# Retention in a fused block: the product with the states takes both heads of a pair at once, from a block-diagonal matrix

## The reference

```python
scores = scale * np.matmul(q, k.transpose(0, 1, 3, 2))      # q, k, v: (4, 8, 576, 64)
Dmat = np.where(rel >= 0, gamma[:, None, None] ** rel[None, :, :], 0.0)
ret = scores * Dmat[None, :, :, :]
attn_out = np.matmul(ret, v)
...
xn = x / rms * rms_g                                        # x: (2304, 512)
g = xn @ w_gate; val = xn @ w_val                           # d_ff 1536
x = (g * (1.0 / (1.0 + np.exp(-g))) * val) @ w_out
...
h = x @ w_in                                                # d_ff 2048
out = np.where(h >= 1, h, np.where(h <= -1, 0.0, (h + 1) ** 2 / 4)) @ w_out2
```

## Time and profile before

| | |
|---|---|
| median of 3 runs | 896.57 us (896.08 to 897.27) |
| the profiled execution, in its own timing | 896.08 us |
| its span, first to last instruction | 894.3 us |
| PE busy | 869.7 us (97% of the span) |
| DVE, ACT, POOL busy | 582.9, 464.6, 204.7 us |
| the retention, until PE's first matmul of step 0 | 91.3 us |

### The profile page before, as it was taken

How to read it: one execution, slowest core, us unless ns; L and a number is a source line. 1 busy time by engine, 2 the same in 40 slices (tenths; PEclk the granted TensorE clock), 3 DMA queues, 4 the chain that set the end, 5 groups by cost and what they waited for, 6 DMA issues and landing times.

```text
span 894.3 us, 17934 instructions
## 1 busy us (share of the span) xinstructions
PE 869.7 (97%) x7448; PEld 850.6 (95%) x7448; DVE 582.9 (65%) x830; ACT 464.6 (52%) x732; POOL 204.7 (23%) x141
## 2 busy tenths in 40 slices
PE   6998999999999999999999999999999999999998
PEld 5887999999999999999999999999999978999998
DVE  3687865577964554632244657857576979978884
ACT  3655654445654555422132347877778846433331
POOL 0324864444864665000033200000000000000000
PEclk9999999999999999999999999999999999999999
DMA  9995133333335434524212004243436573444432
GB/s 266 252 253 117 48 101 101 101 101 100 102 100 190 152 100 158 187 81 159 80 48 80 1 1 154 103 131 130 130 128 223 188 231 119 128 132 120 140 119 71
DMA packets 106991, 114.64 MB, mean 128 GB/s; under 512 B 6592, under 2 KB 81472, under 8 KB 106912
## 3 DMA queue, kind: packets, MB, share of 16 engines
q1 hardware_dynamic: 106912, 113.51, 41.4%
HBM read 75.73 MB, written 37.75 MB: 127 GB/s over the span
## 4 chain that ended last, share of the span: by engine, by line
PE 90%; DVE 4%; ACT 2%; issue 2%; DMA 1%; POOL 1%; SPq 0%; DVEq 0%; ACTq 0%
PE pair L706 16%; PE pair L708 15%; PE pair L707 15%; PE pair L804 6%; PE pair L806 6%; PE pair L805 6%; PE pair L864 5%; PE pair L866 5%; PE pair L865 5%; PE pair L620 2%; PE pair L650 2%; PE pair L656 2%; PE pair L635 1%; PE pair L834 1%; PE pair L836 1%
## 5 line engine op out<-in xcount | busy, mean ns | idle before, releaser
L706 PE MATMUL pair<-xc,wc 128*128 128x288 f32 x672 | 199.4, 297 | 0.6 <-ACT cp L991 0.2
L707 PE MATMUL pair<-xc,wc 128*128 128x288 f32 x672 | 198.2, 295 | 0.0
L708 PE MATMUL pair<-xc,wc 128*128 128x288 f32 x672 | 197.6, 294 | 0.0
L991 ACT ACTIVATE cp<-pair 128x576 f32<-128x576 f32 x160 | 103.4, 647 | 155.1 <-PE pair L708 149.2
L1721 POOL TENSOR_TENSOR wc<-wt,wc 128x512 fp32r<-128x512 f32 x84 | 122.5, 1481 | 92.2 <-ACT wc L923 69.1
L706 PE MATMUL pair<-xc,wr 128*128 128x288 f32 x448 | 132.9, 297 | 0.9 <-ACT cp L991 0.9
L707 PE MATMUL pair<-xc,wr 128*128 128x288 f32 x448 | 132.2, 295 | 0.0
L708 PE MATMUL pair<-xc,wr 128*128 128x288 f32 x448 | 131.7, 294 | 0.0
L706 PEld LDWEIGHTS pair<-xc,wc 128*128 128x128 f32 x672 | 125.9, 187 | 1.6 <-issue 1.5
L708 PEld LDWEIGHTS pair<-xc,wc 128*128 128x128 f32 x672 | 126.5, 188 | 0.0
L707 PEld LDWEIGHTS pair<-xc,wc 128*128 128x128 f32 x672 | 126.1, 188 | 0.0
(11 more groups left out here) (129 smaller groups left out, 1651.0 us busy)
## 6 DMA issues: line engine op xcount, KB each, us to landing
b_scratch<-cb SPq DMA_DIRECT2D x32, 576.0 KB, 2.9
a_scratch<-cb SPq DMA_DIRECT2D x24, 576.0 KB, 2.9
av_r<-a_scratch SPq DMA_DIRECT2D x8, 1728.0 KB, 7.5
wt<-wB SPq DMA_DIRECT2D x72, 128.0 KB, 2.8
bt<-b_scratch SPq DMA_DIRECT2D x28, 256.0 KB, 2.8
bt<-b_scratch SPq DMA_DIRECT2D x56, 128.0 KB, 3.0
a_k<-kT SPq DMA_DIRECT2D x16, 288.0 KB, 8.6
a_q<-qT SPq DMA_DIRECT2D x16, 288.0 KB, 6.9
```

Of the source, the lines that this page charges most:

```text
L706: pe.matmul(o, wh, xh, start=FIRST[i] and j == 0, stop=False, skip_group_check=True)
L707: pe.matmul(o, wh, xl, start=False, stop=False, skip_group_check=True)
L708: mm = pe.matmul(o, wl, xh, start=False, stop=j == 1, skip_group_check=True)
L991: act.activation(copied(g, n)[:, :, :], pair[(X, Q, X, X)[n]][:, :, 0:HALF], ACT.Copy).then_inc(s_c, 1)
```

## The change

The two heads' states are copied into a matrix `a_D` whose other two quadrants are zero: for each chunk 128 x 128, with head 0 in rows and columns 0 to 63, and head 1 in rows and columns 64 to 127. One matmul with it gives both heads, so the second half of `outputs` has 5 matmuls of 128 x 128 weights in place of 10 of 64 x 64. DVE writes the zeros once at the start. POOL fills the diagonal for each pair, in a new function `diagonal(u)`. There is one `a_D`, so `diagonal(u)` waits until `outputs(u-1)` is over. PE's wait for the states moves from ahead of the first half to a wait for `diagonal(u)` ahead of the second half.

```diff
+        a_D = follow("a_D", [NC - 1, P], at, z_a21)
...
-                pe.wait_ge(s_st, (NC - 2) * (u + 1))
-                pe.wait_ge(s_st0, u + 1)
...
+                pe.wait_ge(s_dg, 2 * (u + 1))
                 for c in range(1, NC):
-                    for h in range(2):
-                        rows = slice(HD * h, HD * h + HD)
-                        mm = pe.matmul(b_ob[rows, c // 3, (c % 3) * C:(c % 3 + 1) * C],
-                                       a_S[rows, i, c - 1, :], a_q[rows, p, c, :],
-                                       start=False, stop=True, skip_group_check=True)
+                    mm = pe.matmul(b_ob[:, c // 3, (c % 3) * C:(c % 3 + 1) * C], a_D[:, c - 1, :], a_q[:, p, c, :],
+                                   start=False, stop=True, skip_group_check=True)
...
             def first_state(u):
                 act.wait_ge(s_kv, u + 1)
                 if u > 1:
-                    act.wait_ge(s_ob, u - 1)
+                    act.wait_ge(s_dg, 2 * (u - 1))
...
+            dve.memset(a_D[:, :, :], 0.0).then_inc(s_init, 1)
...
+            def diagonal(u):
+                pool.wait_ge(s_st0, u + 1)
+                pool.wait_ge(s_st, (NC - 2) * (u + 1))
+                if u:
+                    pool.wait_ge(s_ob, u)
+                if u > 1:
+                    pool.wait_ge(s_x, u - 1)
+                for h in range(2):
+                    rows = slice(HD * h, HD * h + HD)
+                    pool.tensor_copy(a_D[rows, :, rows], a_S[rows, u % 2, :, :]).then_inc(s_dg, 1)
+                pool.wait_ge(s_dg, 2 * (u + 1))
+
             pool.wait_ge(d_tab, 80)
+            pool.wait_ge(s_init, N_INIT)
+            diagonal(0)
             for u in range(NA):
+                if u + 1 < NA:
+                    diagonal(u + 1)
```

More of the change, by code:

```diff
@@ L263, in build @@
         s_st = sem("s_st")
+        s_dg = sem("s_dg")
         s_ev = sem("s_ev")
@@ L312, in build @@
         s_od = sem("s_od")
-        N_INIT = 8
+        N_INIT = 9
         block = ctx.enter_context(nc.Block())
```

## The result

| | before | after |
|---|---|---|
| median | 896.30 us (20 executions, 891.56 to 899.85) | 900.11 us (20 executions, 893.41 to 904.29) |
| ratio | | 1.0043 (1.0029 to 1.0057) |
| timed again, later | 895.85 us (23 executions) | 900.57 us (12 executions), ratio 1.0038 (1.0018 to 1.0058) |
| span of the profiled execution | 894.3 us | 897.1 us |
| PE, POOL busy | 869.7, 204.7 us | 873.5, 221.5 us |

The change costs 3.8 us. The forecast was 0.7 us of gain; the time lies inside the range and on the other side of no change.

The account below looks back on a forecast made before the run. Up to us 77 PE and the loads run nose to tail, the loads a little slower. Terms 0 + 0.4 - 1.5 - 1.6 + 2.0 = -0.7 us gave 895.9 us; 8-in-10 range 893.9 to 900.5.

Parts of the forecast that it names:

- `states(14)` at 77.4 doesn't move: Near the retention's end: the start of `states(14)` is set by a landing of loads, so it stays at 77.4; change 0.
- The second half, 1.17: PE's second half of `outputs`: ten weight loads 0.117 apart take 1.17 us, 0.20 more a pair; 1.23 if matmul spacing holds.
- The two longer halves: Retention's end on PE: the longer second halves of `outputs(13)` and `outputs(14)` lose 0.4 us.
- The copies, 0.6 each: POOL's `diagonal(u)`: two copies of 64 partitions x 320 elements at 0.6 us each, with 0.1 for waits 1.3.
- The code packet: PE's stall near us 78, waiting for its next instructions: moves into `outputs(13)`, shrinks to 1.2 us; gain 1.5 (bounds 0.4, 2.7).
- The clock, gain 1.6: PE behind the stall near us 78: the clock stays at full, so `outputs(13)` runs at full speed; gain 1.6 us.
- POOL's tail, +2.0 (bounds 0.8 and 2.9): POOL from the end of `outputs(14)` to low part S2, ahead of sub-product 3: `diagonal(15)` and A11 added; loss 2.0 us.
- (B): Rival at the retention's end, 899 us, chance 0.18: stall and low clock stay as they are, only +0.4 and +2.0 remain.
- (C): Rival on POOL, 901 us, chance 0.12: making its library current now comes behind `diagonal(1)`; beyond 6.6 us each us costs one.
- (A): Rival at the retention's end, 894.1 us, chance 0.18: instruction packet comes in time (1.2 more), copies take 0.3 each (0.6 less).

Follow-up runs that it names:

- the early pairs: New form and its copies in pairs 0 to 13 only, pairs 14 and 15 as in the kernel before: 896.93 us, ratio 0.9984.
- the weights later: New form and copies in pairs 0 to 13 only, and next stage's first weights loaded three pairs later, against the kernel before: 899.72 us, ratio 1.0049.
- the kernel with the low parts first: The changed kernel with the low parts ahead of the copies in POOL's list, each followed by a wait for its end: 897.64 us, ratio 1.0026 to before.
- the third profile of before: The kernel before, unchanged, profiled a third time: 896.55 us.
- the third profile of after: The changed kernel, with no further edit, profiled a third time: 896.04 us.

## Why the prediction was wrong, step by step

**`states(14)` at 77.4 doesn't move.** Open. The profiled execution had 81.3, of which 3.4 are a half clock from 31.4 on; without falls both kernels have 78.7 on average over their profiles, give or take 0.8. It is no longer set by a landing alone: PE needs 0.31 more in each pair, the slack is used up, and the loads follow PE. The executions as a whole point to some cost here: +0.4 ± 0.6 for the early pairs with the packet's gain in it, +1.4 ± 0.5 with the weights later. The term stood at nothing in the sum, and 1.3 to 1.5 is the estimate for it.

**The second half, 1.17.** It is 1.28, above the bound of 1.23, +0.31 in place of +0.20. The pace was right: the loads start 0.111 apart where I took 0.117, and the columns don't set it (1.25 with half of them). What the sum 10 x 0.117 left out is 0.17 us at the two ends of the half, next to matmuls of other shapes. The two longer halves cost 0.6, not 0.4.

**The copies, 0.6 each.** 0.45 as a rule (0.95 for two at 86.16), 0.54 to 1.07 beside those instructions of DVE that have all their operands in SBUF (1.47 for two at 90.36, 2.00 in the kernel with the low parts first). `diagonal(15)` with its waits took 1.76 (90.15 to 91.91) in place of 1.3.

**The code packet.** The place was right: the stall moved to `outputs(13)`, behind its first matmul (2 passes, as forecast), and is 1.29 long (1.2 forecast). The gain in the end of the retention is 1.1 (8.9 to 8.4, with 0.6 for the halves) in place of 1.5.

**The clock, gain 1.6. This step failed.** At its place it came as forecast, the fall near 81 is gone in five profiles of five. But it didn't shorten the time, since the falls come elsewhere: over 32 executions of after and 118 of before the mean clocks are 0.9951 and 0.9956 (± 0.0004 on the difference; a gain of 1.6 us would be +0.0018). What I took for a cost of this place is a cost of the whole program: one kernel pays it near 81 and near 367, the other mostly near 31. The stalls near 31 and 81 move with the packet borders, and each of them can bring a fall.

**POOL's tail, +2.0 (bounds 0.8 and 2.9).** It measured +2.7. Two things were missed. The gate isn't the low part S2 at sub-product 3. It is sub-product 1, by way of ACT: `square(14)` and behind it the rounding of the weights wait for `decay(14)`. And an earlier end of `outputs(14)` is in part given back: `diagonal(14)`, the low part and `decay(13)` bind POOL until then. Where `outputs(14)` ended soonest (7.3 after `states(14)`) the tail is 12.9, where it took 8.9 the tail is 11.6.

**The sum.** Forecast: 0 + 0.4 - 1.5 - 1.6 + 2.0 = -0.7. Measured: 0.6 - 1.1 + 2.7 = +2.2 in the end and the tail by the profiles, and +0.5 ± 0.5 for the clock. The executions give 3.5 clock-free and 4.1 as a mean. What is between 2.2 and 3.5, 1.3 us, the profiles don't place: their own scatter at `states(14)` is 1 us each way. The early pairs are where it would have to be, by the two kernels above (0.4 + 1.1 = 1.5). Of the 4.8 us from -0.7 to 4.1 the clock makes 2.1, the early pairs 1.3, POOL's tail 0.7, the packet 0.4 and the second halves 0.2 (rounded; the part of the early pairs is what the others leave). With the clock alone put right the forecast would have been a loss of 0.9 and not a gain. That the time lies inside the stated range is luck in good part: the range reached up there for (B) and (C), and neither came as it was written.

**The rivals.** (C) fell: the library cost nothing. POOL's timeline of after has the copies of `diagonal(1)` and `decay(0)` back to back (0.08 us between them):

```profile
17.31 0.96 POOL L1756 COPY a_D<-a_S 64x320 f32<-64x320 f32 x2 [2.79 <-PE pair L657]
18.35 1.42 POOL L1715 TENSOR_TENSOR xr<-xr,qdec_s 128x576 f32<-128x576 f32 x1
```

(A) fell with the copies' price: its 0.3 us each isn't met by any copy here, the shortest take 0.44. The Trainium skill, "GPSIMD Engine Reference", section "Engine selection", calls one-input instructions about line rate, from which I had estimated 0.27 us; the measurement decides, and it is 0.44 at the least. (B) gave the nearest time, 899, and its mechanism, read narrowly, isn't what happened, since stall and fall did leave their place. In substance it was right that the clock gives nothing back. I gave it 0.18. The Trainium skill, "TensorE: Matmul & The Clock Gate", section on LDWEIGHTS, gives 107 ns for such a load, and the trace agrees within 5%, with 0.111 us between two of them. And what "TensorEngine Tiling (Array Packing)", section "Key Properties", says of tiles that load in parallel is what this change gives up: twenty small loads and multiplications in 0.97, ten large ones in 1.28. The trace agrees with it.

## What to carry to other kernels

Joining two quarter-array matmuls in one of the whole array halves the instructions and doesn't shorten the time, when the pace is that of the weight loads; it was paid with 0.31 us a pair on PE and up to 2 us of copies in the list of an engine that was the last before the next stage. Don't count a clock fall that goes away at one place as a gain: compare the mean granted clock of many executions, and cost the change on the times without the falls. When a copy is put into an engine's list, follow who waits for each instruction behind it, through other engines' lists too (here ACT's square), and not only for the last one.

## What the runs showed of the hardware that I had not expected

- **The run-to-run scatter of this kernel is mostly the clock.** The time goes from 898.8 to 893.7 us as the mean granted clock goes from 0.992 to 0.998; falls come as pieces of 3.4 or 6.8 us (one of 10.2, one of 13.7) at half clock.
- **The length of a stall doesn't decide on a fall.** A stall of 2.11 us (28.92 in after) was followed by 6.8 us at half clock, one of 2.39 in before by 3.4. The plainest case is the first matmul of `chain_y` (line 804), where PE waits for DVE for 1.91 us in every profile of every version, behind the same work. The clock fell for 3.4 us within 1.5 us of the end of this wait in 9 of 20 profiles, and not in the others. In before it did, in after it didn't (timelines of PE):

```profile
367.27 0.37 PE L804 MATMUL pair<-av,wo 128*128 128x288 f32 x1 [1.91 <-DVE av L1426]
```

```profile
371.04 0.37 PE L804 MATMUL pair<-av,wo 128*128 128x288 f32 x1 [1.91 <-DVE av L1427]
```

  In the third profile of before a stall of 2.50 wasn't followed by any either. Its timeline of PE, and the granted clock behind the stall (stretch of time):

```profile
34.19 0.38 PE L656 MATMUL pair<-a_q,a_S 64*64 64x96 f32 x2
37.06 0.98 PE L656 MATMUL pair<-a_q,a_S 64*64 64x96 f32 x18 [2.50 <-issue]
```

```profile
37.10:45.00 7.90, 7.90 (x170) 6.99 (x171) 4.64 (x9) 5.24 (x9) 2.60 (x2) 1.00 0.98 231
```

  What decides it stays open; no run here was made for it.
- **The same code stalls or not from one execution to the next.** The changed kernel stood still for 2.1 to 2.6 us near 30 in three of five profiles, and in another had no gap from 22.3 to 78.8.
- **A copy of 64 x 320 on POOL takes 0.45 us, and up to 1.07 beside some of DVE's work.** It isn't DVE's being busy that counts. The second copy of the two at 86.16 has DVE's mask beside it, which reads PSUM, and takes 0.45. The one at 90.96 has a sum beside it that reads and writes SBUF alone, and takes 0.87. So it is with all copies of after: 0.44 or 0.45 beside masks or nothing, 0.54 to 0.99 where `xt`, `xc` or `wt` are made meanwhile. DVE's timeline at the first place, DVE's at the second, and POOL's there:

```profile
86.67 0.75 DVE L1266 TENSOR_TENSOR a_r<-pair,mask_s 96x576 f32<-96x576 f32 x1 [0.77 <-PE pair L623]
```

```profile
90.52 1.00 DVE L1342 TENSOR_TENSOR xt<-xr 128x576 f32<-128x576 f32 x1
```

```profile
90.96 0.87 POOL L1756 COPY a_D<-a_S 64x320 f32<-64x320 f32 x1
```

- **The half clock at the start is in no mean.** `PEclk` is 1.00 in these profiles from the first microsecond, but `scores(0)` takes 2.23 or 2.24 us in all 20, where 1.26 is the time at full clock (behind the fall at 31.4 it was 2.17 in the chain). The first full-speed work comes at 14 to 22 us, at other times in other executions. In the third profile of after it comes last (timeline of PE, then the stretch of time):

```profile
20.32 2.07 PE L623 MATMUL pair<-a_q,a_k 64*96 64x96 f32 x24
```

```profile
4.00:22.00 18.00, 12.98 (x142) 11.99 (x144) 5.49 (x13) 5.42 (x10) 2.21 (x5) 1.00 1.02 250
```
